# Second head's q and k loaded beside the first's, and the steps around the last projection and the router made in another order

## The reference

```python
# q, k, v: (2, 8, 1152, 64)
q_pool = q.reshape(B, H, S // 2, 2, D).mean(axis=3)
scores = scale * np.matmul(q_pool, k.transpose(0, 1, 3, 2))
attn = np.exp(scores - np.max(scores, axis=-1, keepdims=True))
attn = attn / (np.sum(attn, axis=-1, keepdims=True) + 1e-09)
attn_out = np.matmul(attn, v)                  # (2, 8, 576, 64)
x = attn_out.transpose(0, 2, 1, 3).reshape(1152, 512)
# gated projection, 512 -> 1536 -> 512
gate = 1.0 / (1.0 + np.exp(-(x @ w_gate)))
x = gate * (x @ w_val) @ w_out
# mixture: router (512, 8), w1 (8, 512, 1024), w2 (8, 1024, 512)
logits = x @ router
P = np.exp(logits - logits.max())
for _ in range(8):
    P /= P.sum(1, keepdims=True) + 1e-09
    P /= P.sum(0, keepdims=True) + 1e-09
    P *= N / E
for e in range(E):
    out += P[:, e:e + 1] * (np.maximum(x @ w1[e], 0.0) @ w2[e])
```

## Time and profile before

| | |
|---|---|
| time, median of 3 runs (lowest, highest) | 1298.61 us (1298.49, 1298.71) |
| profiled execution: time, span | 1297.78 us, 1296.0 us |
| mean granted PE clock | 0.997 of 2.4 GHz |
| busy in the span | PE 98%, weight loads 90%, DVE 60%, ACT 46%, POOL 44% |
| DMA | 84.85 MB, mean 65 GB/s |

### The profile page before, as it was taken

One profiled execution on the slowest core, in us unless ns is written; L12 is line 12 of the kernel. 1 busy time (PEld: TensorE's weight loads), 2 busy tenths in 40 slices (PEclk: granted clock), 3 DMA queues, 4 the chain that ended last, 5 costly groups with the idle time before them and its releaser, 6 DMA issues.

```text
span 1296.0 us, 20394 instructions
## 1 busy us (share of the span) xinstructions
PE 1273.6 (98%) x7800; PEld 1167.5 (90%) x7800; DVE 783.0 (60%) x1728; ACT 602.5 (46%) x1321; POOL 572.3 (44%) x356
## 2 busy tenths in 40 slices
PE   7999999999999998899999999999999999999999
PEld 6999999889999988898999899899998999999997
DVE  7999999983222323657656656556556465466443
ACT  7999899883333333344434334334333233234221
POOL 6377777761121346354425325335335245245211
PEclk9999999999999999899999999999999999999999
DMA  5334334202111133122222222123122122122112
GB/s 138 58 69 74 71 66 73 51 10 74 49 32 32 58 98 98 33 65 66 60 71 67 65 66 81 50 65 98 36 80 82 50 81 66 49 82 72 46 47 90
DMA packets 104091, 84.85 MB, mean 65 GB/s; under 512 B 14016, under 2 KB 80576, under 8 KB 104000
## 3 DMA queue, kind: packets, MB, share of 16 engines
q1 hardware_dynamic: 103856, 83.33, 23.8%
q10 hardware_dynamic: 144, 0.29, 0.1%
HBM read 79.15 MB, written 2.40 MB: 63 GB/s over the span
## 4 chain that ended last, share of the span: by engine, by line
PE 91%; DVE 5%; POOL 1%; ACT 1%; DMA 1%; issue 0%; SPq 0%; POOLq 0%
PE bank L915 10%; PE bank L917 10%; PE bank L916 10%; PE bank L1057 10%; PE bank L1058 10%; PE bank L1059 10%; PE bank L758 6%; PE bank L777 5%; PE bank L892 4%; PE bank L894 4%; PE bank L893 4%; PE bank L786 3%; PE bank L787 3%; DVE part_min L1371 1%; PE bank L751 1%; PE bank L744 1%
## 5 line engine op out<-in xcount | busy, mean ns | idle before, releaser
L1485 DVE TENSOR_TENSOR c<-bank,c 128x256 f32<-128x256 f32 (+1 forms) x448 | 197.3, 457 | 290.9 <-PE bank L917 282.4
L695 POOL TENSOR_TENSOR w_lo<-w_raw,w_hi 128x1024 fp32r<-128x1024 f32 x64 | 154.1, 2408 | 303.9 <-ACT w_hi L1074 303.9
L1058 PE MATMUL bank<-w_lo,h_hi 128*128 128x512 f32 x576 | 224.8, 390 | 0.0
L1057 PE MATMUL bank<-w_hi,h_hi 128*128 128x512 f32 x576 | 224.8, 390 | 0.0
L1059 PE MATMUL bank<-w_hi,h_lo 128*128 128x512 f32 x576 | 224.1, 389 | 0.0
L1240 ACT ACTIVATE h_hi<-c 128x256 fp32r<-128x256 f32 (+1 forms) x256 | 112.6, 445 | 168.8 <-DVE c L1485 168.3
L1059 PEld LDWEIGHTS bank<-w_hi,h_lo 128*128 128x128 f32 x576 | 108.2, 188 | 23.0
L1371 DVE TENSOR_REDUCE part_min<-bank 128x1 f32<-128x256 f32 (+2 forms) x240 | 122.1, 555 | 11.2 <-PE bank L787 8.2
L1057 PEld LDWEIGHTS bank<-w_hi,h_hi 128*128 128x128 f32 x576 | 108.2, 188 | 20.8
L1058 PEld LDWEIGHTS bank<-w_lo,h_hi 128*128 128x128 f32 x576 | 108.2, 188 | 20.1
L1074 ACT ACTIVATE c<-bank 128x256 f32<-128x256 f32 (+1 forms) x64 | 26.3, 412 | 212.8 <-PE bank L917 212.8
(11 more groups left out here) (153 smaller groups left out, 3135.8 us busy)
## 6 DMA issues: line engine op xcount, KB each, us to landing
w_raw<-in_moe_w SPq DMA_DIRECT2D x64, 512.0 KB, 3.7
w_raw<-in_moe_w SPq DMA_DIRECT2D x64, 256.0 KB, 3.0
wo_raw<-in_moe_w_out SPq DMA_DIRECT2D x16, 384.0 KB, 3.5
v_raw<-in_v SPq DMA_DIRECT2D x16, 288.0 KB, 3.3
k_raw<-in_k SPq DMA_DIRECT2D x15, 288.0 KB, 8.3
q_raw<-in_q SPq DMA_DIRECT2D x16, 256.0 KB
gv_raw<-in_moe_w_gate SPq DMA_DIRECT2D x12, 256.0 KB, 2.9
gv_raw<-in_moe_w_val SPq DMA_DIRECT2D x12, 256.0 KB, 3.2
```

The source lines that it names most:

```text
L695: nc.gpsimd.tensor_tensor(w2_lo[:, u % 2], w2_raw[:], f32(w2_hi[:, u % 2]), ALU.subtract).then_inc(w2_split, 1)
L1057: nc.tensor.matmul(bank[:, 3 + i], hh, wh, start=first, stop=False)
L1058: nc.tensor.matmul(bank[:, 3 + i], hh, wl, start=False, stop=False)
L1485: nc.vector.tensor_tensor(dst[:, 0:w], bank[:, (u + b) % 3, 0:w], other[:, 0:w], ALU.add).then_inc(done, 1)
```

## The change

1. Head 1 gets buffers of its own, `q_first` and `k_first`. Its q is loaded by SP behind head 0's q and ahead of v, its k by ACT's queue behind head 0's k, all at the start. The loads of `gv_raw` and the router, which lay behind head 1's, move behind head 3's. The buffers lie where `gv_raw` lies later.
2. POOL: `wo_lo_part(6)` moves ahead of the two `t_lo_part(0, ...)`, `wo_lo_part(7)` ahead of `w2_lo_part(0)`. SP: `load_wo(7)` moves ahead of `load_w1(1)`. ACT: `xf_part(5)` moves ahead of `wo_hi_part(7)`.
3. The last projection step, k = 7, goes through its chunks once, both halves at each chunk. In its middle it signals `h1_half_read`, and ACT makes the whole of w1's block 1 then (its place in SBUF is moved so that only the first chunks lie there), ahead of `x_hi(7)`.
4. DVE: of `t_sums(1)` the first sum is made after step 5, the other three move from ahead of `w1_sums(3)` to behind `hidden_sums(1)` and the logits.
5. ACT: block 3 of w1 is made between the copies of the router's result, ahead of `p1_copy(1)`; it stood behind `hidden(1)`.
6. Router: the `_hi` and `_lo` weights of each chunk lie side by side (16 rows of result instead of 8), so the lo·hi matmul is left out: 24 matmuls instead of 36. DVE adds the two parts: the copy and the maximum become a copy, an addition and a maximum.
7. ACT: with `w1_hi_part` of later experts split, `y_copies` stands between its raw pieces and its sums.

```diff
@@ sync @@
             load_q(0)
+            load_q(1)
             load_v(0)
-            sp.wait_ge(q_summed, 2)
-            sp.wait_ge(k_split_done, 1)
-            load_kq(1)
-            load_gv(0, 0)
-            load_gv(1, 1)
-            sp.dma_start(router_raw[:], router_dram).then_inc(router_loaded, 16)
...
+                if h == 1:
+                    load_gv(0, 0)
+                    load_gv(1, 1)
+                    sp.dma_start(router_raw[:], router_dram).then_inc(router_loaded, 16)
...
             load_w1(2)
+            load_wo(2 * DCH - 1)
             load_w1(1)
-            load_wo(2 * DCH - 1)
@@ gpsimd @@
             w1_lo_part(0)
+            wo_lo_part(DCH + 2)
             t_lo_part(0, 0)
             t_lo_part(0, 1)
-            wo_lo_part(DCH + 2)
+            wo_lo_part(DCH + 3)
             w2_lo_part(0)
-            wo_lo_part(DCH + 3)
...
             w1_lo_part(2)
+            w1_lo_part(3)
             w2_lo_part(1)
-            w1_lo_part(3)
+            w2_lo_part(2)
             t_lo_part(1, 0)
             t_lo_part(1, 1)
-            w2_lo_part(2)
@@ tensor, last projection step @@
+                if k == 2 * DCH - 1:
                     for f in range(F1CH):
+                        chunk(0, f)
+                        chunk(1, f)
@@ tensor, router @@
-                        mm = split_product(bank[:, 3 + b, 0:BLK], router_hi[:, sl], router_lo[:, sl],
-                                           x2(x_hi, c, b), x2(x_lo, c, b), c == 0, c == DCH - 1)
+                        nc.tensor.matmul(bank[:, 3 + b, 0:BLK], weights, x2(x_hi, c, b), start=(c == 0), stop=False)
+                        mm = nc.tensor.matmul(bank[:, 3 + b, 0:BLK], weights, x2(x_lo, c, b), start=False, stop=(c == DCH - 1))
@@ scalar @@
             act.dma_start(k_raw[:], k_dram[0]).then_inc(k_loaded, 16)
+            act.dma_start(k_first[:], k_dram[1]).then_inc(k_first_loaded, 16)
...
                 if n == 1 and e < NEXP - 1:
-                    w1_hi_part(MCH * (e + 1) + m)
+                    w1_hi_raw(MCH * (e + 1) + m)
                 if u in (MCH, 2 * MCH):
                     y_copies(u // MCH - 1)
+                if n == 1 and e < NEXP - 1:
+                    w1_hi_sums(MCH * (e + 1) + m)
@@ vector @@
             hidden_sums(0)
-            t_sums(1)
             w1_sums(3)
             hidden_sums(1)
...
+            nc.vector.tensor_tensor(logit_te, by_part[:, :, 1], logit_te, ALU.add).then_inc(logit_copied, 1)
+            dve.wait_ge(logit_copied, 2)
+            nc.vector.tensor_reduce(lmax[:, 0:1], logit[:], AX.X, ALU.max).then_inc(lmax_done, 1)
+            t_sums_others(1)
```

More of the change, by code:

```diff
@@ L100, in build @@
                 ("lmax", [PARTS, 3], F32)])
+        with ExitStack() as s:
+            k_first, _, q_first = allocate(s, [
+                ("k_first", [PARTS, KCH, DIM], F32),
+                ("k_first_to", [PARTS, 2 * DCH * PARTS - KCH * DIM], F32),
+                ("q_first", [PARTS, QT, 2 * DIM], F32)])
         gv_raw0, gv_raw1, gv_hi0, gv_lo0 = allocate(ctx, [
@@ L177, in build @@
                     ("w1_lo0", [PARTS, 14, PARTS], F32R)])
-                TB_hi, TB_lo, w1_hi1, w1_lo1, w1_hi2, w1_lo2, w1_hi3, w1_lo3 = allocate(over, [
+                w1_hi1, w1_lo1, TB_hi, TB_lo, w1_hi2, w1_lo2, w1_hi3, w1_lo3 = allocate(over, [
+                    ("w1_hi1", [PARTS, 14, PARTS], F32R),
+                    ("w1_lo1", [PARTS, 14, PARTS], F32R),
                     ("TB_hi", [PARTS, DCH, 2 * WIDE[1]], F32R),
                     ("TB_lo", [PARTS, DCH, 2 * WIDE[1]], F32R),
-                    ("w1_hi1", [PARTS, 14, PARTS], F32R),
-                    ("w1_lo1", [PARTS, 14, PARTS], F32R),
                     ("w1_hi2", [PARTS, 14, PARTS], F32R),
@@ L348, in all_heads, with pool_q @@
                 head(h, h // 2, h % 2)
-        def pool_q(engine, a):
+        def pool_q(engine, a, src, done):
             for rows, tiles in ((PARTS, slice(0, 4)), (QROWS[4], slice(4, 5))):
                 wide = [rows, tiles.stop - tiles.start, 2, DIM]
-                first = q_raw[0:rows, tiles, 0:DIM].unsqueeze(2).to_broadcast(wide)
-                second = q_raw[0:rows, tiles, DIM:2 * DIM].unsqueeze(2).to_broadcast(wide)
-                engine.tensor_tensor(q_sum[a][0:rows, tiles], first, second, ALU.add).then_inc(q_summed, 1)
+                first = src[0:rows, tiles, 0:DIM].unsqueeze(2).to_broadcast(wide)
+                second = src[0:rows, tiles, DIM:2 * DIM].unsqueeze(2).to_broadcast(wide)
+                engine.tensor_tensor(q_sum[a][0:rows, tiles], first, second, ALU.add).then_inc(done, 1)
         def scores(j):
@@ L1146, in _ @@
             act.dma_start(k_raw[:], k_dram[0]).then_inc(k_loaded, 16)
+            act.dma_start(k_first[:], k_dram[1]).then_inc(k_first_loaded, 16)
             act.wait_ge(k_loaded, 16)
-            copy(k_split[0][:, :, 0], k_raw[:]).then_inc(k_hi_done, 1)
+            copy(k_split[0][:, :, 0], k_raw[:]).then_inc(k_hi_done[0], 1)
             for t in range(QT):
@@ L1285, in _, with logitT_copy @@
                     w2_hi_part(0)
+            def logitT_copy(b):
+                act.wait_ge(logitT_ready, b + 1)
+                copy(logitT[:, b * BLK:(b + 1) * BLK], bank[0:2 * NEXP, 3 + b, 0:BLK]).then_inc(logitT_done, 1)
             hi_11(0)
-            w1_hi_sums(1)
             hi_others(0)
             w1_hi_part(2)
-            for b in range(NBLK):
-                act.wait_ge(logitT_ready, b + 1)
-                copy(logitT[:, b * BLK:(b + 1) * BLK], bank[0:NEXP, 3 + b, 0:BLK]).then_inc(logitT_done, 1)
+            logitT_copy(0)
+            w1_hi_raw(3)
+            logitT_copy(1)
+            logitT_copy(2)
+            w1_hi_sums(3)
             for u in range(1, NUNIT):
```

153 lines of the change are left out of this document (91 added, 62 removed).

## The result

The changed kernel took 1287.15 us (median of 4 runs, 1286.37 to 1287.76) against 1298.66: a ratio of 0.9911 (95% interval 0.9894 to 0.9928). The forecast was 1288.6, its range 1286.0 to 1291.5. The profiled execution took 1286.37 us, span 1284.6, 11.4 less than the span of before.

A forecast was written before the change was run, and what follows sets the result against it. PE bounds the kernel, busy 1273.6 of 1296.0 us. The terms -0.8 - 3.7 - 2.1 - 1.9 - 1.5 = -10.0 took the median of 1298.61 to 1288.6 us; range 1286.0 to 1291.5.

The forecast's parts named there:

- the rival in which the clock is kept: In hidden(1) the wait is too short for a clock fall or DVE gets in first: -11.8, 1286.8 us; chance 0.25.
- the fall of the clock in hidden(1): PE's clock falls at the 2.6 us wait in hidden(1), taken as likelier, at a price of 1.8 us.
- the slip: At the start, POOL's first addition goes ahead and attention starts 1.2 later: 1.4 to 2 us more, 1290.3; chance 0.2.
- Start and attention: Start and head 1: early operands -0.2, head 0's q landing later +0.5, shorter den -1.1; together -0.8 us.
- the 1.1 of the sum: Head 1: POOL is done with head 3's k earlier, so DVE's den addition falls from 1.42 to 0.17; 1.1 us gained.
- Nothing changes for later heads: Attention after head 1: POOL's order is tied to PE's, so nothing changes there.
- Steps 6 and 7: Projection: both waits, 1.91 and 1.79 us, go because wo_lo is ready earlier; -3.70 us.
- Router and hidden(1): Router: 12 fewer matmuls, -2.1 us; hidden(1): a shorter wait of 2.6 us stays, -1.9 us by itself.
- the order of turns between DVE and POOL: hidden(1): POOL's pieces and DVE's four w1 sums alternate, the third behind POOL's long piece; sums done at 535.0 us.
- Unit 5: Unit 5: earlier y_copies let p1_copy(5) end about 1.5 us earlier, so PE's wait goes; -1.46 us.
- a sign of being wrong: hidden(2): a wait for c because TB_hi stands ahead of p1_copy(2) would show the prediction wrong.

The follow-up runs named there:

- e6: The kernel before with only the early loads of head 1's q and k into their own buffers: 1300.43 us, ratio 1.0000 to before.
- e1: The changed kernel with its start undone, head 1's q and k loaded behind head 0's as before: 1288.98 us, ratio 0.9907 to before.
- e4: The kernel before with the router part alone, 24 matmuls instead of 36: 1301.06 us, ratio 0.9996 to before.
- e9: The kernel before with only the order of wo changed on SP, POOL and ACT: 1296.22 us, ratio 0.9968 to before.
- e5: The changed kernel itself, measured again with nothing changed: 1289.89 us, ratio 0.9917 to before.
- e8: The changed kernel with four ACT moves: head 1's k load later, p1_copy(1) earlier, TB_hi and the router's exponential later: 1283.55 us, ratio 0.9870 to before.
- e11: The changed kernel with ACT's y_copies back behind all of w1's next block, raw and sums: 1290.09 us, ratio 0.9919 to before.
- e3: The changed kernel with the sums over xfB back ahead of w1's block 3 on DVE: 1294.30 us, ratio 0.9948 to before.
- e7: The changed kernel with ACT's p1_copy(1) ahead of w1_hi_sums(3): 1288.34 us, ratio 0.9909 to before.
- e12: The changed kernel with 14 extra transposes filling PE's wait ahead of head 0's second tile: 1288.76 us, ratio 0.9916 to before.
- e2: The changed kernel with ACT issuing head 1's k load behind its copy of head 0's k: 1286.83 us, ratio 0.9895 to before.

## Why the prediction was right

**The total** was right by terms that were off in both directions. Against the predicted -10.0 the two profiles give -11.4. The median, 1287.15, is nearer to the rival in which the clock is kept (1286.8) than to the forecast (1288.6), and by its mechanism it is that rival: the fall of the clock in hidden(1), a premise of the forecast, didn't happen. That the forecast came so near is in part luck, since 3.2 us too little in hidden(1) stood against 1.7 us of new waits that I hadn't counted. The range also had a wrong end: the slip as I priced it (1.4 to 2) gives 1290.0 to 1290.6, not 1291.5.

**Start and attention: -0.8 predicted, -0.13 in this pair, nothing that can be measured in e6.** q came later by 0.80, the upper end, where I took 0.5. The early operands gave nothing in the end: the scores of tile 1 began 0.71 later than before (12.23, 11.52), and from PE's next transposes on everything was 0.81 later. Then the short `den` gave 1.05, nearly the 1.1 of the sum: the next reduction began at 29.61, and in before it is

```profile
29.85 1.48 DVE L1371 TENSOR_REDUCE part_min<-bank 128x1 f32<-128x256 f32 x3
```

But the step that led to the 1.1 failed. I had POOL done with head 3's k at 27.5, some 3 us earlier. POOL did begin earlier, then it waited 2.70 us for PE's transposes, and its last piece of that k ran from 27.67 to 29.10 (28.02 to 29.43 in before). POOL was still there, and `den` ended within 0.05 us of that piece in both. In before `den` began 0.04 us behind the piece's start and so took 1.42; in the ten profiles with the new loads it began 1.18 to 1.21 behind it and took 0.25 to 0.28. With the old loads it took 0.26, 0.27 and 0.30 in e1, e4 and e9, so the 1.42 that I built on was the exception among four profiles. "Nothing changes for later heads" failed too: a long `den` stands in a later head in e1 (1.75), in e4 (1.65) and in e5, the changed kernel itself (1.50), each time until a piece of POOL's ended.

**Steps 6 and 7: -3.70 predicted, -4.16 measured**, in the changed kernel and in e9 alike. The cause was right, the size short by 0.23 for each wait. PE's matmuls are pipelined (listed with 0.28 us each, they start 0.12 apart), and a listed wait begins at the modelled end of the last one. In the changed kernel and in e8, the same place in hidden(3):

```profile
556.35 0.28 PE L934 MATMUL bank<-TA_hi,w_lo 128*128 128x256 f32 x1
557.19 0.39 PE L932 MATMUL bank<-x_hi,w_hi 128*128 128x256 f32 x1 [0.56 <-ACT c L1103]
557.42 0.28 PE L933 MATMUL bank<-x_lo,w_hi 128*128 128x256 f32 x1
```

```profile
554.37 0.28 PE L934 MATMUL bank<-TA_hi,w_lo 128*128 128x256 f32 x1
554.49 0.28 PE L932 MATMUL bank<-x_hi,w_hi 128*128 128x256 f32 x1
554.61 0.28 PE L933 MATMUL bank<-x_lo,w_hi 128*128 128x256 f32 x1
```

From start to start over two steps 1.07 us against 0.24: a wait listed as 0.56 costs 0.83. e11 shows it too (1.46 listed, 1.69 paid).

**Router and hidden(1): -2.1 and -1.9 predicted, together -4.0; measured -7.15.** The router took 4.18 us, as said. In hidden(1) the mechanism was right (ACT's sums of block 3 ahead of `c`, released by a `w_sum` that POOL stretched), the size not: 1.09 instead of 2.6. The step that failed is the order of turns between DVE and POOL. DVE's third sum got in before POOL's long piece (529.50, 530.14), only the fourth waited (2.50), and the sums were done at 533.0 instead of 535.0. The clock was kept, so that 1.8 more came in: the rival with chance 0.25 happened at this place. The two terms can't be had apart, as I listed them: e4 gives 0 for the router alone, e3 23.0 us for everything but the move of the sums, and all together 16.2. What the other moves in this stretch are worth by themselves, those of w1's blocks 1 and 3 on ACT and of POOL's pieces, no run shows.

**Unit 5: -1.46 predicted, -1.69 by e11.** Right, with the same 0.2 as above.

**What I had not counted: +1.73.** hidden(2) and hidden(3) wait 0.66 and 0.56 for `c`. The rows of the changed kernel, ACT for both and PE for the first:

```profile
544.31 1.27 ACT L1103 ACTIVATE TB_hi<-xfB 128x1280 fp32r<-128x1280 f32 x1 [0.44 <-DVE xfB L1503]
545.49 0.36 ACT L1103 ACTIVATE c<-bank 128x256 f32<-128x256 f32 x1
...
545.91 0.39 PE L932 MATMUL bank<-x_hi,w_hi 128*128 128x256 f32 x1 [0.66 <-ACT c L1103]
...
556.51 0.35 ACT L1345 ACTIVATE weight<-logit,lmax 128x72 f32<-128x72 f32 x1 [4.85 <-DVE lmax L1642]
```

I had named the first as a sign of being wrong, and put `TB_hi` to 547 and the need to 548.8. Both came earlier (545.6 and 545.3), PE more so, since hidden(1) waited less and kept its clock. The second stands behind the router's exponential, which waited 4.85 us for DVE's `lmax` and which I had left out. So the last stretch is where it was (747.24 for 747.20): new waits took what unit 5 gave.

Ledger, changed against before: -0.13 - 4.16 - 7.15 + 0.04 = -11.4.

**Open.** Why the first stretch ends anywhere between 445.9 and 451.4. Where it is decided can be read: by the starts of the 16 `den` additions each profile keeps its distance to the changed kernel's first one within 0.15 us from the eighth on (149 us); all of the spread is made ahead of that. What stands there is q's landing (4.71 to 6.18), the slow transposes (1.0 to 1.4 us), the fall of the clock around 12 to 16 us in e1, e4 and e7, and a long `den` in a later head, behind which e1, e4 and e5 were 1.3, 0.8 and 0.7 us later. Besides, DVE began a reduction late in e5, as against the changed kernel's first profile (shown first):

```profile
74.31 1.52 DVE L1412 TENSOR_REDUCE part_min<-bank 128x1 f32<-128x256 f32 x3 [0.19 <-PE bank L804]
```

```profile
77.15 1.49 DVE L1412 TENSOR_REDUCE part_min<-bank 128x1 f32<-128x256 f32 x3 [1.40 <-PE bank L804]
```

Its first piece waits only for the first 256 columns of scores. They ended at 74.27 in the one and at 75.90 in the other, so DVE came 0.04 us after them here and 1.25 there. PE's wait of 0.90 for `pT_lo` (79.48) follows from it, and with the long `den` it makes the 1.9 us that e5 loses between 58 and 107 us. e12 has the same at 129.99, 2.18 us after its scores, and PE waits 1.83. What held DVE the traces don't tell. Whether e8's small spread is its own or luck of four runs is open too.

## What to carry to other kernels

Before you add up the terms of a change, ask of each whether the same wait ends it: PE work left out ahead of a wait is worth nothing until the chain that ends the wait is shortened. When a wait goes, look at the next instructions of the releasing queue, one unit on: here the next unit's `c` had 1.8 us of cover by the times that I had worked out, and none in the trace. Before you bank a gain from a collision of two engines, see in more than one profile of the old kernel that they collide there. Cut profiles at marks of the bounding engine and compare stretches; that told 0.1 us where whole times spread by 5.

## What the runs showed of the hardware

A second transfer of 288 KB on another engine's queue made the one in flight land at 5.6 to 6.2 instead of 4.7 to 5.0 us; issued at 3.99 (e2) or 4.37 (e8) it cost nothing. A DVE addition that met a piece of POOL's lasted until that piece ended, within 0.05 us, in five profiles (0.26 to 1.75 us for the same `den`).

PE's clock fell in or behind every wait of 2.58 to 6.4 us in these profiles. Behind shorter ones it mostly stayed, but not always: behind 1.78 to 1.80 us ahead of tile 1 it fell to 0.50 in e7 and stayed in five others; behind 1.91 us in step 6 it fell to 0.50 in e4 and e6 and stayed in before. So the length of the wait alone doesn't decide. The price of the fall in hidden(1) was 1.8 us in before and 2.2 in e3; in e4 and e6 0.9 more came behind project(0), where the clock was still low.
